# A fused attention and two-MoE kernel: later normalisations, query copies, first weight loads and two queue positions moved

## The reference

```python
# 1. attention, q/k/v [2, 8, 768, 64]; 4 sink keys, window of 128
scores = (q @ k.T) / sqrt(64)
keep = (pos_k < 4) | ((0 <= pos_q - pos_k) & (pos_q - pos_k < 128))
a = exp(where(keep, scores, -1e9) - max); a = a / (sum(a) + 1e-9)
x = (a @ v) as [1536, 512]
# 2. four experts, w1 [4, 512, 1024], w2 [4, 1024, 512]
p = domain_probs / (sum(domain_probs) + 1e-9)
x = sum_e p[:, e] * (relu(x @ w1[e]) @ w2[e])
# 3. w_in [512, 2048], w_out [2048, 512]
h = x @ w_in;  out = (h * cos(h)) @ w_out
```

## Time and profile before

| | |
|---|---|
| median of three runs | 851.24 us (850.83 to 852.79) |
| the profiled execution | 851.39 us |
| its span | 849.7 us |
| mean granted clock of TensorE | 0.998 of full |
| TensorE busy | 835.3 us, 98% |
| VectorE, ScalarE, GpSimd busy | 462.6, 457.5, 546.4 us |

### The profile page before, as it was taken

How to read it: one execution, slowest core, us unless ns; L and a number is a source line. 1 busy time by engine, 2 the same in 40 slices (tenths; PEclk the granted TensorE clock), 3 DMA queues, 4 the chain that set the end, 5 groups by cost and what they waited for, 6 DMA issues and landing times.

```text
span 849.7 us, 13625 instructions
## 1 busy us (share of the span) xinstructions
PE 835.3 (98%) x4590; PEld 746.1 (88%) x4590; DVE 462.6 (54%) x951; ACT 457.5 (54%) x983; POOL 546.4 (64%) x413
## 2 busy tenths in 40 slices
PE   9998899999999999999999999999999999999998
PEld 6776789989989988988988998998898998898996
DVE  6888633433533527533533433338757758846756
ACT  6697534334334336423423423526867869767863
POOL 4699776566466775675475475876384399585450
PEclk9999999999999999999999999999999999999999
DMA  9983221311211320321131121120230230520202
GB/s 170 237 184 87 88 100 50 100 50 50 100 51 51 98 77 24 100 100 34 67 99 33 69 100 50 50 100 17 84 100 5 96 100 0 175 99 6 94 1 75
DMA packets 73155, 67.29 MB, mean 79 GB/s; under 512 B 40608, under 2 KB 46848, under 8 KB 73088
## 3 DMA queue, kind: packets, MB, share of 16 engines
q1 hardware_dynamic: 72032, 66.16, 25.8%
q10 hardware_dynamic: 1056, 0.26, 0.2%
HBM read 62.96 MB, written 3.19 MB: 78 GB/s over the span
## 4 chain that ended last, share of the span: by engine, by line
PE 87%; POOL 6%; DVE 2%; issue 2%; DMA 1%; SPq 0%; ACT 0%; POOLq 0%; DVEq 0%
PE scores L1360 10%; PE scores L1364 10%; PE scores L1362 10%; PE scores L1392 10%; PE scores L1390 10%; PE scores L1388 10%; PE bank L1390 5%; PE bank L1392 5%; PE bank L1388 5%; PE bank L1360 3%; PE bank L1362 3%; PE bank L1364 3%; POOL weights_t L508 1%; POOL weights_t L511 1%; DVE x_lo L1022 1%
## 5 line engine op out<-in xcount | busy, mean ns | idle before, releaser
L585 POOL TENSOR_TENSOR w_lo<-w_raw,w_hi 128x512 fp32r<-128x512 f32 x96 | 128.5, 1347 | 173.8 <-ACT w_hi L711 173.7
L1360 PE MATMUL scores<-x_hi,w_hi 128*128 128x384 f32 x528 | 178.5, 338 | 1.9 <-ACT kept L750 1.8
L1364 PE MATMUL scores<-x_hi,w_lo 128*128 128x384 f32 x528 | 177.2, 336 | 0.0
L1362 PE MATMUL scores<-x_lo,w_hi 128*128 128x384 f32 x528 | 177.1, 335 | 0.0
L592 POOL TENSOR_TENSOR w_lo<-w_raw,w_hi 128x1024 fp32r<-128x1024 f32 x48 | 116.2, 2430 | 65.1 <-ACT w_hi L721 65.1
L721 ACT ACTIVATE w_hi<-w_raw 128x1024 fp32r<-128x1024 f32 x48 | 50.8, 1059 | 188.6 <-PE scores L1392 188.6
L1392 PE MATMUL scores<-w_hi,h_lo 128*128 128x512 f32 x384 | 149.8, 390 | 0.0
L1390 PE MATMUL scores<-w_lo,h_hi 128*128 128x512 f32 x384 | 149.7, 390 | 0.0
L1388 PE MATMUL scores<-w_hi,h_hi 128*128 128x512 f32 x384 | 149.4, 389 | 0.0
L1121 DVE SCALAR_TENSOR_TENSOR acc<-scores,probs,acc 128x512 f32<-128x512 f32 x56 | 41.8, 749 | 116.5 <-PE scores L1392 116.5
L1360 PEld LDWEIGHTS scores<-x_hi,w_hi 128*128 128x128 f32 x528 | 99.7, 189 | 4.4 <-issue 3.8
(11 more groups left out here) (129 smaller groups left out, 1555.1 us busy)
## 6 DMA issues: line engine op xcount, KB each, us to landing
w_raw<-in_moe_w_dram SPq DMA_DIRECT2D x32, 1024.0 KB, 5.1
w_raw<-in_moe_w_in_dram SPq DMA_DIRECT2D x8, 1024.0 KB, 5.0
w_raw<-in_moe_w_out_dram SPq DMA_DIRECT2D x8, 1024.0 KB, 5.3
v_nat<-in_v_dram SPq DMA_DIRECT2D x12, 256.0 KB, 3.4
norm<-routing_dram SPq DMA_DIRECT2D x24, 128.0 KB, 3.0
out_dram<-acc SPq DMA_DIRECT2D x12, 256.0 KB, 4.0
k_nat<-in_k_dram SPq DMA_DIRECT2D x11, 256.0 KB, 4.0
q_nat<-in_q_dram SPq DMA_DIRECT2D x11, 256.0 KB, 4.5
```

Source lines behind the costliest of these rows:

```text
L585: nc.gpsimd.tensor_tensor(w1_slots(w1_lo, h % 2, part), w1_part(h % 2, part), w1_slots(w1_hi, h % 2, part).bitcast(F32), ALU.subtract)\
L1360: nc.tensor.matmul(target[:, 0:HALF], w1_hi[:, i, slot, d], x_hi[:, n - 1, d], start=first and d == 0, stop=False, skip_group_check=True)
L1362: nc.tensor.matmul(target[:, 0:HALF], w1_hi[:, i, slot, d], x_lo[:, n - 1, d], start=False, stop=False, skip_group_check=True)
L1364: last = nc.tensor.matmul(target[:, 0:HALF], w1_lo[:, i, slot, d], x_hi[:, n - 1, d], start=False, stop=d == 1, skip_group_check=True)
```

## The change

- Tiles 5 to 11 of x are normalised by VectorE (`NORM_BY_DVE = 5`): tiles 5 to 8 in rounds 16, 18, 20 and 22, between `invert_sums` and the next round; tiles 9 and 10 in round 26; tile 11 in stage 0 behind its last `relu_lo`, ahead of `keep_down`. GpSimd keeps tiles 0 to 4, and its loop ends with round 26.
- The turned queries of tiles 6 to 11 are copied by ScalarE (`QUERIES_BY_ACT = 6`), behind the fourth exponential of rounds 10, 12, ... 20, instead of by VectorE.
- The first stage's w1 and w2 come in four loads of 256 KB each: w1 in SyncE's passes 1 to 4, w2 in passes 5 to 8, each behind `load_norm`. GpSimd's first weight sums move from rounds 7 to 10 to rounds 9 to 12, its low parts from 12 to 17 to 14 to 19, ScalarE's high parts from 11 to 16 to 13 to 18. The waits count four landings for the first stage's weights.
- The first halves of keys and queries are all issued by SyncE, in the order keys, queries, keys, queries; before, ScalarE issued the queries'.
- `turn_sinks(T - 1)` stands behind products 2 and 6 of round 25.
- In the two stages that open a gated block, `keep_2(b)` stands ahead of the whole turns `n + 1` and `n + 2` instead of behind their folds.

```diff
+NORM_BY_DVE = 5
+QUERIES_BY_ACT = 6
...
-            load_half(sp, k_nat, k, 0, first_landed[0])
-            load_half(sp, k_nat, k, 1, k_landed[0])
+            load_half(k_nat, k, 0, first_landed[0])
+            load_half(q_nat, q, 0, first_landed[1])
+            load_half(k_nat, k, 1, k_landed[0])
+            load_half(q_nat, q, 1, q_landed[0])
...
+            def load_part(dst, n, part, signal):
+                sp.dma_start(dst[:, part], weights_of(0)[n][part * P:(part + 1) * P, :]).then_inc(signal, 16)
...
-                if t == 2:
-                    load_first(0)
-                if t == 4:
-                    load_second(0)
                 if 0 <= t - 2 < T:
                     load_norm(t - 2)
+                if t <= KC:
+                    load_part(w1_raw, 0, t - 1, w1_landed)
+                elif t <= 2 * KC:
+                    load_part(w2_raw, 1, t - KC - 1, w2_landed)
...
-                    pool.wait_ge(w1_landed, 16 * (s + 1))
+                    pool.wait_ge(w1_landed, 16 * (s + KC))
...
-            for i in range(ROUNDS + 3):
+            for i in range(ROUNDS):
...
-                if 7 <= i < 11:
-                    sum_weights(0, i - 7)
-                if 12 <= i < 18:
-                    first_lo(*divmod(i - 12, 3))
-                if i % 2 == 0 and 0 <= (i - 6) // 2 < T:
+                if 9 <= i < 13:
+                    sum_weights(0, i - 9)
+                if 14 <= i < 20:
+                    first_lo(*divmod(i - 14, 3))
+                if i % 2 == 0 and 0 <= (i - 6) // 2 < NORM_BY_DVE:
                     normalise((i - 6) // 2)
...
+            def copy_queries(t):
+                act.wait_ge(q_turned, t + 1)
+                act.wait_ge(scores_done, PAIRS * (t - 1))
+                nc.scalar.activation(q_t[:, t % 2], turn_bank[:].rearrange("p (k s) -> p k s", k=PAIRS), ACT.Copy)\
+                    .then_inc(q_ready, 1)
...
-            load_half(act, q_nat, q, 0, first_landed[1])
-            load_half(act, q_nat, q, 1, q_landed[0])
...
+                if i % 2 == 0 and QUERIES_BY_ACT <= i // 2 + 1 < T:
+                    copy_queries(i // 2 + 1)
...
-                if 11 <= i < 17:
-                    first_hi(*divmod(i - 11, 3))
+                if 13 <= i < 19:
+                    first_hi(*divmod(i - 13, 3))
...
-                    if not opens(s):
+                    if opens(s):
+                        keep_2(b)
+                    else:
                         keep_1(b)
                     whole(n + 1)
                     whole(n + 2)
                     fold(n + 1)
                     fold(n + 2)
-                    keep_2(b)
+                    if not opens(s):
+                        keep_2(b)
...
+            def normalise(t):
+                dve.wait_ge(x_ready, t)
+                dve.wait_ge(x_copied, t + 1)
+                dve.wait_ge(norm_landed[t % 2], 32 * (t // 2 + 1))
+                g, i = divmod(t, TPB)
+                tile = x_t[:, g, :, i * P:(i + 1) * P]
+                nc.vector.tensor_tensor(tile, tile, norm[:, t % 2], ALU.mult).then_inc(x_ready, 1)
...
-                elif i % 2 == 0 and i // 2 + 1 < T:
+                elif i % 2 == 0 and i // 2 + 1 < QUERIES_BY_ACT:
                     copy_queries(i // 2 + 1)
                 if i % 2 == 0 and 0 <= (i - 2) // 2 < T:
                     invert_sums((i - 2) // 2)
+                if i % 2 == 0 and i < ND and (i - 6) // 2 >= NORM_BY_DVE:
+                    normalise((i - 6) // 2)
...
+                if i == ND + 2:
+                    normalise(T - 3)
+                    normalise(T - 2)
...
                     relu_lo(b, 21)
+                if s == 0:
+                    normalise(T - 1)
...
-                if i % 2 == 1 and 0 <= (i - 3) // 2 < T:
+                if i % 2 == 1 and 0 <= (i - 3) // 2 < T - 1:
                     turn_sinks((i - 3) // 2)
...
                 if i == ND + 1:
                     product(0, 2)
                     product(0, 6)
+                    turn_sinks(T - 1)
```

More of the change, by code:

```diff
@@ L285, in heads @@
             return src[b, :, i * P:(i + 1) * P, :].rearrange("h s d -> s h d")
-        def load_half(engine, dst, src, n, signal):
-            half = H // 2
-            engine.dma_start(dst[:, 0, n * half * D:(n + 1) * half * D].rearrange("p (h d) -> p h d", h=half),
-                             heads(src, 0)[:, n * half:(n + 1) * half]).then_inc(signal, 16)
         def sums_in_memory(t):
@@ L359, in _, with load_half @@
         def _(sp):
+            def load_half(dst, src, n, signal):
+                half = H // 2
+                sp.dma_start(dst[:, 0, n * half * D:(n + 1) * half * D].rearrange("p (h d) -> p h d", h=half),
+                             heads(src, 0)[:, n * half:(n + 1) * half]).then_inc(signal, 16)
             def load_keys(t):
@@ L714, in second_hi @@
             def second_hi(s, i):
-                act.wait_ge(w2_landed, 16 * (s + 1))
+                act.wait_ge(w2_landed, 16 * (s + KC))
                 if s >= 1 and i == 0:
```

6 lines of the change are left out of this document (2 added, 4 removed).

## The result

The changed kernel takes 861.64 us (median of four runs, 860.58 to 863.21), the kernel before 852.01 beside it (850.83 to 854.07): ratio 1.0112, 95% interval 1.0084 to 1.014. It is slower by 9.6 us. The prediction said 849.8 us and a range of 845.3 to 853.0; it was wrong, in sign and in size. The 9.6 us are a net figure: one part of the change, the later turn of the last sinks, gains some 4.2 us (run 7), so the rest costs about 14. The profiled execution took 860.92 us with a span of 859.2 (before 851.39 and 849.7).

The account below looks back on a forecast made before the run. The prediction took TensorE's gaps as the bound, with GpSimd busy 55.4 of 56 us in attention. Terms 2.0 - 4.2 + 0.85 = -1.4 us (rounded); 851.39 - 1.4 - 0.15 = 849.8 us, range 845.3 to 853.

Parts of the forecast that it names:

- Normalisations of tiles 9 and 10 now stand before VectorE's first addition ... no gap (ends 0 and +1.5): After round 25: addition made at 99.5 us, TensorE reaches product 4 at 99.6, so no gap.
- Some 0.35 for GpSimd's operation under way: Tile 5's normalisation in round 16: VectorE's delay from a running GpSimd operation, 0.35 us, counted once.
- the second rival: VectorE becomes the bound: normalisations of tiles 6, 7, 8 each cost 1.2 us more, 3.6 in all; 853.4 us, chance 0.12.
- Term: +2.0: Round 16: VectorE waits 1.8 us for tile 5's norm and starts round 17 some 2.2 us later; ends 0 and 3.2.
- I count 0 in rounds 18 and 20: Tiles 6 to 8: norm and VectorE meet within half a us, so no loss in these rounds.
- +0.8: Round 22's normalisation stands before the first token split and round 23's masks; the gap at 85.39 grows; ends 0 and 1.6.
- So the fourth part goes at about 37.9 ... I take 3.4: 41.3 us (ends 40.8 and 42.5): First weights' fourth load: issued about 37.9, landing 41.3 us; GpSimd waits, TensorE's step at 43.27 barely moves, +0.05.
- GpSimd's stand at 41 us swallows it: 0: Start: first loads sharing SyncE's queue delay it +0.4, at most +1.0 us; counted as 0 net.
- Round 19, "-1.5": The 1.54 us gap of TensorE at the sinks in round 19 goes, a gain of 1.5 us.
- The tail, "-4.2": Last sinks turned later: round 25's 2.84 us gap and 1.4 us of low clock go; ends -4.4 and -1.5.
- The kept copy, "+0.85": Gated openings: product 5's waits close, product 3 waits for L757, net 0.85 us slower; ends -1.8 and +1.3.
- Rival 1: Relief whole: VectorE finds norms landed; gaps of rounds 19, 23, 25 close; about 846.3 us as middle, chance 0.34.

Follow-up runs that it names:

- run 7: The kernel before, with only the last sinks' turn moved behind products 2 and 6 of round 25: 847.49 us, ratio 0.9948.
- run 5: The changed kernel with one more wait: GpSimd holds the second weights' low parts (L601) until tiles 9 and 10 are normalised: 856.74 us, ratio 1.0058.
- run 1: The changed kernel with tiles 9, 10 and 11 normalised by GpSimd again, tiles 5 to 8 still by VectorE: 855.91 us, ratio 1.0047.
- run 2: The changed kernel with all twelve normalisations on GpSimd, the change's other parts kept: 852.97 us, ratio 1.0026.
- run 3: The changed kernel with the first stage's weights in one load each, their sums, high and low parts in their old rounds: 859.12 us, ratio 1.0089.
- run 10: Run 9 with tiles 5 to 8 normalised by VectorE, weights whole, tiles 9 to 11 on GpSimd waiting for tile 8: 852.36 us, ratio 1.0011.
- run 9: Run 8 with the query copies of tiles 6 to 11 moved to ScalarE: 847.18 us, ratio 0.9938.
- run 6: The changed kernel with VectorE multiplying tiles 5 to 8 by a constant tile, without the norm loads' wait (SyncE waits instead): 858.13 us, ratio 1.0076.
- run 4: The changed kernel with the kept copy back behind the folds: 858.5 us, ratio 1.0091.
- run 8: Run 7 with the kept copy, in the two stages opening a gated block, between the whole turns and their folds: 846.01 us, ratio 0.9932.
- run 11: Run 8 with VectorE's first two token splits one round later: 846.6 us, ratio 0.993.
- run 12: Run 11 with GpSimd's four token sums one round later, behind the gathering of the sinks: 849.01 us, ratio 0.9964.

## Why the prediction was wrong

**The step that failed most: "Normalisations of tiles 9 and 10 now stand before VectorE's first addition ... no gap (ends 0 and +1.5)".** The step counted 0.9 us for each product and found product 4 just in time, at 99.6. It looked at VectorE's queue alone. GpSimd's two operations of 2.4 us, the low parts of the second weights, run at the same time. Beside them the products take 2.87 and 2.8 us, which costs a gap of 3.43 and a low stretch of about 1.6 us: 5 us where the term had 0. Run 5 shows it with nothing but a wait (4.6 us less), run 1 with the products moved (4.9 less). The trace of before had what was needed: the split of 1.98 instead of 0.91.

**"Some 0.35 for GpSimd's operation under way", once.** Undersized. The Trainium skill ("SBUF — State Buffer", Who interferes with whom) says that whichever starts first holds the port for its whole length and the other blocks. By that the sum would have been 1 to 2 us higher in the rounds. The trace agrees: GpSimd's sum at 78.46 ends at 80.27, and VectorE's product, begun at 78.68, ends 0.55 later, a little less than the 0.68 that it takes alone; GpSimd's next cast then takes 0.70 us (0.24 elsewhere). Of the 1.42 us that TensorE waits for what follows this explains 0.5; the rest is GpSimd's own queue, with the first weights' low parts in it: in run 2, which has them in the same rounds, and no normalisation on VectorE, the gap is 2.49, and in run 3, which has them earlier, there is none. The prediction knew the rule, had the row, and put it into the second rival at 1.2 us each for tiles 6, 7, 8; it should have gone into the sum, and have been asked of every GpSimd operation that the moved product can meet. Rival 2 was the right mechanism, and still 8 us too low in total: it gave rounds 16 to 23 3.6 us more and the tail nothing.

**"Term: +2.0" for tile 5, "I count 0 in rounds 18 and 20", "+0.8" for rounds 22 to 24.** The norm wait at tile 5 came as worked out: VectorE stands (1.32 us after a start that is already late, 1.98 in run 10). The sum of the rounds did not: round 24's part begins 6.5 us late, not 2.0. Of this 2.8 us were there by round 13 (0.75 predicted), 0.72 is a norm wait at tile 8, where none was counted, 1.42 is the gap of round 21, which the sum did not have, and the rest is tile 5 and the meetings with GpSimd, less the 1.4 of round 19. The shares do not add up: VectorE's four tiles without the late weights cost 4.5 us by there (run 10), the late weights without VectorE's tiles about 4 (run 2 against run 9), both together 6.5. In the same way the norm wait and the meetings stand in for one another (run 6).

**"So the fourth part goes at about 37.9 ... I take 3.4: 41.3 us (ends 40.8 and 42.5)".** It went at 38.17 and let GpSimd start at 42.63, at the upper end. That put 0.96 us on the gap of round 11, and a low stretch followed, about 1.6 more: the term of +0.05 measured 2.5 in this profile. In the profiles of runs 1, 2 and 4 a gap of 1.92 to 2.20 us stands in its place with full clock behind it, so that there it is about 1. Round 13's own +0.7 did not show here, and came out as a gap of 0.63 or 0.64 in those three. Run 3 gets 3.1 us back at 47 us and 1.7 in the end.

**"GpSimd's stand at 41 us swallows it: 0" (start).** The start came 0.84 late, above the taken 0.4 and inside the ends. The other profiles with these loads have the scores of round 2 at 11.02 to 11.30 us instead of 11.67, those with the old loads at 10.75 to 11.19, so a good part of it is scatter. By round 11 more than half was swallowed.

**Round 19, "-1.5".** Right: the gap is gone, 1.44 us came back.

**The tail, "-4.2".** Right for the moved turn itself: run 7 gives 4.2 us, run 2 4.3. In the changed kernel the gap of 2.84 is gone, and the clock's 1.4 were not earned, since a low stretch follows the gap of 3.01 us at 91.87.

**The kept copy, "+0.85".** Right, with the wait where it was said to be: product 3, for L757 (now L772), 1.31 us at each opening against 0.59 and 1.18 before, 0.85 more in all, of which 0.8 show in the lateness of the last matmul. The price is for the place ahead of the whole turns; one place later, behind them, the same copy is a gain (run 8: 1.5 us with the medians compared).

**The clock** was a term of the sum only where the change removed a gap. It was not asked what a new gap would do. In the changed kernel's profile the three gaps of 2.05, 3.01 and 3.43 us were each followed by a stretch at 1.2 GHz that cost 1.6 us: 8.5 us of standing became 13.3. No run gives a length of gap from which this happens (see the last section).

The bound of "about 11 us" on the gain holds: the best version took 5.7 of it. Rival 1 (846.3) is close to this time by luck only: relief of GpSimd has no part in run 8, where it is busy 55.4 of 56 us. What stays open is how the 6.5 us by round 23 divide between the late weights, the norm waits and the meetings, and how much of each time is the clock's scatter.

## What to carry to other kernels

A product of two SBUF tensors that is moved from GpSimd to VectorE takes its own time only where no GpSimd operation is under way; list the GpSimd operations that it can meet, and add up to their whole length, for the later one stands behind the earlier, and its engine's queue behind it. A step that waits for a DMA costs most on an engine whose next steps others wait for, however idle that engine is on average (run 10: 1.98 us of waiting ahead of the next round's maxima). Look first for work that only has to stand behind something else in TensorE's order: one such move (run 7) gave 4.2 us, and its profile has full clock and no new gap at the products behind it.

## What the runs showed of the chip that was not expected

- The run's time follows the mean clock: 852.3 us at 0.999 and 858.54 at 0.992 in run 1, 852.38 at 1.0 and 860.43 at 0.988 in run 5. After a gap of 3.0 us the lower level lasted 3.4 us in one profile and some 10 in another, TensorE being fully busy in both. The length of the gap does not decide alone whether the clock falls: behind a gap of 1.65 us in round 18 it fell within 0.6 us in run 1's profile, and behind 1.92 and 2.20 us in round 11 it stayed full in those of runs 4, 1 and 2. Runs 7, 8, 9 and 11, whose profiles have no gap above 1.9 us in attention, had a mean clock of 0.999 or 1.0 and scattered by 2.2 us at most; run 12 has none above 1.6 us, yet scattered by 3.7 us, with 0.996 in two of six runs.
- A small operation loses as much as a large one: the TENSOR_SCALAR of 8 columns took 1.81 us at 70.23, and ended 0.03 us after GpSimd's sum, which had started 0.03 us before it. The kernel before has this too, up to 1.15 us; the twelve take 5.7 us there, 7.4 in the changed kernel and 5.8 in run 2.
- One wait more on GpSimd made the changed kernel 4.6 us faster (run 5) and GpSimd's own pair 0.6 us shorter.
